# Padding rows issued by one queue instead of two, and 128-column matmuls for half-filled expert tiles

## The chip, the cores and the metric

The kernel runs on one core of a Trainium2 chip. A core has TensorE (matmuls, into PSUM), VectorE, ScalarE, GpSimd and SyncE, each with its own stream of instructions, and 16 DMA engines that serve the queues of SyncE, ScalarE and GpSimd. The engines meet only at semaphores. The metric is the time of one execution on the device, in microseconds.

## The reference

Three stages, each of which takes what the one before gives:

```python
# 1: attention over channels: q, k, v are [2, 5056, 256]
qn = q / (norm(q, axis=1) + 1e-6);  kn = k / (norm(k, axis=1) + 1e-6)
a = softmax(kn.transpose(0, 2, 1) @ qn / tau)          # 256 x 256 per batch
x = (v @ a).reshape(10112, 256)

# 2: mixture of experts, top 1 of E = 8, F = 1024
logits = normalized(x) @ normalized(expert_emb).T / moe_tau
e = argmax(logits);  gate = softmax(logits)[e]
x = gate * (maximum(x @ w1[e], 0) @ w2[e])

# 3: a second one, with its own weights and a second gate
logits = x @ w_gate
e = argmax(logits);  gate = softmax(logits)[e]
out = gate * sigmoid(x @ w_output_gate)[e] * (maximum(x @ w1_b[e], 0) @ w2_b[e])
```

How many tokens an expert gets depends on the data.

## The kernel before

Each of the five engines has one program, written out by hand as a block of the function below.

**Attention.** q and k are loaded in 16 units, TensorE multiplies them (L1116), ScalarE squares them for the norms, whose sums TensorE makes against ones (L1125, L1128). Then v is transposed (L1144) and multiplied with a (L1168), two 128-token slots at a time, with 264 columns: 256 channels and 8 expert logits. VectorE copies the result into `arena` (L847) and works out for every token its expert and its place in that expert's region.

**Dispatch.** GpSimd scatters each row into the DRAM buffer `xbuf[0]` (L503), where expert e has a region of its own from row e·CAP. After the last row of a region there may be old data in the last tile that is read. So `pad_regions` writes 256 pad rows (gate 0, an id that no token has) behind each expert's rows: it loads the expert's count from `plan` (L339) and issues one transfer of 264 KB (L341). There are 8 experts in each of the two layers. SP pads the even experts and ScalarE the odd ones. SP then waits for all scatters (L434, L437) and for all pads (L439), and only then loads the first tile (L443).

**The two expert layers** (m = 0 and 1) run the same loop, `each_tile`, on every engine: over the experts, two at a time, over the full tiles of 256 tokens, and then one tail tile if the count rounded up to 128 is odd. The tail's `subs` is 1, that of a full tile 2. In each tile TensorE does:

- first matrix (L1233): eight chunks c of 128 hidden channels, each 2 × 3 matmuls in reduced-precision fp32 (fp32r): weights are split in a high and a low part, and so is x, and three of the four products are made. The moving operand is x, transposed, with `tok` columns;
- transposes of the next tile's x (L1190);
- second matrix (L1249): per 128 tokens 24 matmuls with 256 columns. It waits for h.

ScalarE evicts each chunk with Relu into `h_hi` (L722) and VectorE makes `h_lo` (L1048), both only over the `subs` × 128 columns that hold tokens. PSUM has four buffers for the chunks. Layer 0 has more in its tiles: TensorE transposes the previous tile's y (L1197), makes its logits (L1204, 16 columns, full fp32) and its ranks (L1210, L1211), VectorE routes it, and GpSimd scatters it into `xbuf[1]`.

The weights of the next expert are split while the current one runs. Where an expert has only a tail tile, the pieces of the split are put between the evictions of that tile: ScalarE's high parts at L624 and L629, VectorE's low parts at L821 and L828, GpSimd's at L520.

Of the tail tile, TensorE's program says before the change:

```python
tok = SUB * P                  # 256, also where subs is 1
... T.matmul(h_ps(c, tok), w1_halves[w][:, par, d, c * P:(c + 1) * P], x_halves[x][:, d, :], ...)
```

so in a tail tile columns 128 to 255 are computed from the rows behind the tile's tokens, and nobody reads them.

Of the kernel before, what the change touches and what calls it, by code (L numbers as in the profile page):

```python
# [28 lines left out]
P = 128  # L29


def build(nc, q, k, v, tau, emb, moe_tau, w1_a, w2_a, w_gate, w_ogate, w1_b, w2_b, out):
    B, N, C = q.shape
    TOK = B * N
    E, _, FF = w1_a.shape
# [14 lines left out]
    SUB = 2  # L50
    PADROWS = SUB * P
    CAP = TOK + PADROWS
# [4 lines left out]
    xbuf = [nc.dram_tensor(f"dispatched_{m}", [E * CAP, ROW], F32, kind="Internal").ap() for m in range(2)]  # L57
# [3 lines left out]
    with ExitStack() as ctx:  # L61
# [19 lines left out]
        pad_rows = sb("pad_rows", [P, SUB, ROW])  # L81
# [93 lines left out]
        plan = [sb(f"plan_{m}", [P, 2, E], I32) for m in range(2)]  # L175
# [19 lines left out]
        def h_ps(c, t):  # L195
            return ps[:, c % HRING, 0:t]
# [48 lines left out]
        padded = [sem(f"padded{m}") for m in range(2)]  # L245
# [87 lines left out]
            eng.dma_start(w1_raw[:, r, :, :], w1_d[m][e]).then_inc(raw_in[r], 16)  # L333
            eng.dma_start(w2_raw[:, r, :, :], w2_d[m][e]).then_inc(raw_in[r], 16)

        def pad_regions(eng, m, first):

            for e in range(first, E, 2):
                count = eng.value_load(plan[m][0:1, 0, e:e + 1], min_val=0, max_val=TOK)  # L339
                dst = xbuf[m][bass.ds(count + e * CAP, PADROWS), :]  # L340
                eng.dma_start(dst.rearrange("(p s) r -> p (s r)", s=SUB), pad_rows[:, :, :].rearrange("p s r -> p (s r)")).then_inc(padded[m], 16)  # L341

        def each_tile(eng, m, before_expert, body, tile, next_weights=None):


# [41 lines left out]
        @block.sync  # L387
        def _(sp):
            def load_group(dst, src, g, signal):

                rows = src[0:FULL * P, :].rearrange("(p t) c -> p t c", t=FULL)
                if g % 2 == 0:
                    sp.dma_start(dst.rearrange("p (t c) -> p t c", c=C), rows[:, g * G:(g + 1) * G, :]).then_inc(signal, 16)
                    return
                body = dst[:, 0:(G - 1) * C].rearrange("p (t c) -> p t c", c=C)
                sp.dma_start(body, rows[:, g * G:(g + 1) * G - 1, :]).then_inc(signal, 16)
                if g < NG - 1:
                    sp.dma_start(dst[:, (G - 1) * C:], rows[:, (g + 1) * G - 1, :]).then_inc(signal, 16)
                else:
                    sp.dma_start(dst[0:REST, (G - 1) * C:], src[FULL * P:N, :]).then_inc(signal, 16)  # L400

            def load_unit(dst, src, j, signal):

                rows = src[0:FULL * P, :].rearrange("(p t) c -> p t c", t=FULL)
                m = U if j < NU - 1 else U - 1
                sp.dma_start(dst[:, 0:m * C].rearrange("p (t c) -> p t c", c=C), rows[:, j * U:j * U + m, :]).then_inc(signal, 16)
                if m < U:
                    sp.dma_start(dst[0:REST, m * C:], src[FULL * P:N, :]).then_inc(signal, 16)

            for n in range(B * NU):  # L410
                b, j = divmod(n, NU)
                if n >= QRING:
                    sp.wait_ge(qk_multiplied, n - QRING + 1)
                    sp.wait_ge(qk_squared, n - QRING + 1)
                load_unit(qk[:, n % QRING, 0, :], q[b], j, qk_in[n % QRING])
                load_unit(qk[:, n % QRING, 1, :], k[b], j, qk_in[n % QRING])
            for n in range(B * NG):
                b, g = divmod(n, NG)
                if n == 2:
                    sp.wait_ge(norm_done, B)  # L420
                    load_weights(sp, 0, 0, 0)
                if n >= 2:
                    sp.wait_ge(vt_done, PAIRS * (n - 1))
                load_group(v_sb[:, n % 2, :], v[b], g, v_in[n % 2])
                if n == 2:
                    load_weights(sp, 0, 1, 1)

            tile = sp.alloc_register("sp_tile")
            for m, L in enumerate(layers):
                sp.wait_ge(plan_ready, m + 1)  # L430
                pad_regions(sp, m, 0)
                if m == 0:
                    for g in range(NG):
                        sp.wait_ge(scattered[g], 16 * G * B)  # L434
                else:
                    n_end = sp.snap(tile)
                    hold(sp, layers[0].y_scattered, n_end * 16 * SUB)  # L437
                    hold(sp, layers[0].xT_ready, n_end + 1)
                sp.wait_ge(padded[m], 16 * E)  # L439

                def load_tile(n, row):
                    hold(sp, L.xT_ready, n)
                    sp.dma_start(x_in[:, :, :], xbuf[m][bass.ds(row, SUB * P), :].rearrange("(s p) r -> p s r", p=P)).then_inc(L.x_in, 16)  # L443

                def body(n, subs, pair, par, t):
                    load_tile(n, pair * (2 * CAP) + par * CAP + t * (SUB * P))

                each_tile(sp, m, lambda *a: None, body, tile)
                load_tile(sp.snap(tile), 0)
            hold(sp, layers[1].y_scattered, sp.snap(tile) * (16 * SUB))  # L450
# [122 lines left out]
        def _(act):  # L573
# [120 lines left out]
            tile = act.alloc_register("act_tile")  # L694
            for m, L in enumerate(layers):
                act.wait_ge(plan_ready, m + 1)
                pad_regions(act, m, 1)
                take_xT(L, 1)

                def before_expert(pair, par, n):  # L700

                    hold(act, w1_split, 2 * pair + (E * m + par + 1))
                    hold(act, w2_split, 2 * pair + (E * m + par + 1))
                    hold(act, w2_split_dve, 2 * pair + (E * m + par + 1))
                    with act.If(pair < E // 2 - 1):
                        load_weights(act, m, nc.s_assert_le(2 * pair + (2 + par), E - 2 + par), par)
                    if m == 0:
                        with act.If(pair > E // 2 - 2):
                            load_weights(act, 1, par, par)

                def ahead(pair, par, n):

                    hold(act, layers[m].tile_done, n)
                    unless_last(act, m, pair, par, lambda: split_w2_hi(pair + (E // 2 * m + par), 1 - par))

                def behind(pair, par, first):
                    unless_last(act, m, pair, par, lambda: split_w1_hi(pair + (E // 2 * m + par), 1 - par))

                def body(n, subs, pair, par, t, splitting=False):
                    for c in range(FC):  # L720
                        act.wait_ge(L.h_done[c], n)
                        nc.scalar.activation(h_hi[:, c, 0:subs * P], h_ps(c, subs * P), ACT.Relu).then_inc(L.h_hi[c], 1)  # L722
                        if m == 0 and c == (3 if subs == 1 else 2):
                            take_yT(n)
                        if splitting:
                            piece = w1_piece if c < WPIECES else w2_piece
                            unless_last(act, m, pair, par, lambda: piece(pair + (E // 2 * m + par), 1 - par, c % WPIECES))
                    take_xT(L, n + 1)
                    if m == 0:
                        y_exps(n)  # L730

                each_tile(act, m, before_expert, body, tile, (ahead, behind))
                if m == 0:
                    n_end = act.snap(tile)
                    take_yT(n_end)
                    y_exps(n_end)
# [345 lines left out]
        def _(pe):  # L1082
            T = nc.tensor
# [132 lines left out]
            for m, L in enumerate(layers):  # L1216
# [6 lines left out]
                    pe.wait_ge(w1_split, pair * 2 + (E * m + par + 1))  # L1223

                def body(n, subs, pair, par, t):
                    tok = SUB * P
                    pe.wait_ge(L.xT_ready, n + 1)
                    for c in range(FC):
                        if c >= HRING:
                            pe.wait_ge(L.h_ready[c - HRING], n)  # L1230
                        for d in range(CC):
                            for at, (w, x) in enumerate(PARTS):
                                last = T.matmul(h_ps(c, tok), w1_halves[w][:, par, d, c * P:(c + 1) * P], x_halves[x][:, d, :],  # L1233
                                                start=(d == 0 and at == 0), stop=(d == CC - 1 and at == len(PARTS) - 1))
                        last.then_inc(L.h_done[c], 1)
                        if m == 0 and c == (2 if subs == 1 else 1):
                            transpose_y(n)
                        if m == 0 and c == (5 if subs == 1 else 4):
                            y_logits(n)
# [46 lines left out]
```

## Time and profile before

| | |
|---|---|
| median of 3 runs | 1494.57 us (1494.0 to 1497.95) |
| the profiled execution | 1497.95 us |
| its span, first to last instruction | 1496.2 us |
| mean granted TensorE clock | 0.934 of full speed |
| tiles | 46 in layer 0, 45 in layer 1 |
| layer 0 / layer 1 begin (first matmul of L1233) | 281.75 / 949.62 us |

TensorE's matmuls overlap: the time that one is shown to last is longer than the distance to the next, so the sum over a group is more than it costs. The clock is 1.00 where TensorE runs at 2.4 GHz and 0.50 where it runs at 1.2 GHz. "PEld" is TensorE's weight load, which goes ahead of each matmul. In the timeline and the chain, an entry with x18 stands for 18 instructions in a row. Full fp32 matmuls appear as two records each, fp32r matmuls and transposes as one.

### The profile page before, as it was taken

Reading aid. Unit: us, or ns where it says so; the run is one execution under the profiler, and the core shown is the slowest. Engines: PE = TensorE matmul, PEld = TensorE weight load, DVE = VectorE, ACT = ScalarE, POOL = GpSimd, SP = SyncE. Lnnn points to the kernel's source line nnn. Section 1 sums busy time; section 2 is a strip of 40 time slices with the busy share of each in tenths; the row PEclk is TensorE's granted clock in tenths of the full one; section 3 lists DMA queues with packets and bytes.
Section 4 is the critical chain, followed back from the end, with each engine's and each line's share of the span. In section 5 each row is a group of like instructions: output and inputs, shape, how many; then the busy total and the mean of one; then the engine's idle time right before and its main releaser. Section 6 shows DMA issues by size and latency. Waiting matters only on the chain.

```text
span 1496.2 us, 30926 instructions
## 1 busy us (share of the span) xinstructions
PE 1327.4 (89%) x10518; PEld 1302.1 (87%) x10519; DVE 805.6 (54%) x2751; ACT 550.5 (37%) x1339; POOL 384.0 (26%) x510
## 2 busy tenths in 40 slices
PE   8978562499999997899999976699999999999985
PEld 7867562499999997899999975699999999999985
DVE  5457455356555567656555566344444544444584
ACT  6547454233333344333333343222333332223362
POOL 1002455312222123312222123222222222222343
PEclk9989686699999998999999987799999999999998
DMA  8635422411111124211111142411111211111260
GB/s 315 244 123 197 142 104 88 156 36 36 43 43 43 36 93 135 82 40 36 43 43 43 36 129 78 144 50 43 43 43 49 94 48 44 48 43 43 96 204 16
DMA packets 68766, 126.20 MB, mean 84 GB/s; under 512 B 9044, under 2 KB 49887, under 8 KB 67712
## 3 DMA queue, kind: packets, MB, share of 16 engines
q1 hardware_dynamic: 35600, 62.57, 13.4%
q10 hardware_dynamic: 20368, 31.55, 6.2%
q0 software_dynamic: 12768, 31.74, 5.9%
q8 instruction: 11, 0.18, 0.1%
q14 instruction: 19, 0.16, 0.0%
HBM read 89.79 MB, written 39.90 MB: 87 GB/s over the span
## 4 chain that ended last, share of the span: by engine, by line
PE 80%; DVE 7%; issue 4%; another core or an unknown queue 2%; ACT 2%; DMA 1%; SPq 1%; DVEq 0%; ACTq 0%; POOL 0%; POOLq 0%
PE ps L1233 35%; PE ps L1249 30%; PE ps L1116 5%; PE ps L1204 3%; PE ps L1190 2%; DVE w_lo L828 2%; PE ps L1168 2%; PE ps L1197 2%; DVE arena L847 1%; DVE h_lo L842 1%; PE ps L1144 1%; ACT w_hi L629 1%; DVE xT_lo L950 0%; DVE w_lo L821 0%
## 5 line engine op out<-in xcount | busy, mean ns | idle before, releaser
L722 ACT ACTIVATE h_hi<-ps 128x256 fp32r<-128x256 f32 (+1 forms) x728 | 268.0, 370 | 694.4 <-PE ps L1233 684.8
L1233 PE MATMUL ps<-xT_hi,w_hi 128*128 128x256 f32 x1456 | 428.1, 294 | 26.2 <-issue 10.8
L1048 DVE SCALAR_TENSOR_TENSOR h_lo<-ps,h_hi 128x256 fp32r<-128x256 f32 (+1 forms) x728 | 294.1, 405 | 245.6 <-ACT h_hi L722 222.6
L1233 PE MATMUL ps<-xT_lo,w_hi 128*128 128x256 f32 x1456 | 415.5, 285 | 0.0
L1233 PE MATMUL ps<-xT_hi,w_lo 128*128 128x256 f32 x1456 | 415.2, 285 | 0.0
L1249 PE MATMUL ps<-w_hi,h_hi 128*128 128x256 f32 x1352 | 393.2, 291 | 0.0
L1249 PE MATMUL ps<-w_lo,h_hi 128*128 128x256 f32 x1352 | 381.8, 282 | 0.0
L1249 PE MATMUL ps<-w_hi,h_lo 128*128 128x256 f32 x1352 | 381.6, 282 | 0.0
L1233 PEld LDWEIGHTS ps<-xT_hi,w_hi 128*128 128x128 f32 x1456 | 284.1, 195 | 30.5 <-issue 17.9
L1233 PEld LDWEIGHTS ps<-xT_hi,w_lo 128*128 128x128 f32 x1456 | 283.2, 194 | 0.0
L1233 PEld LDWEIGHTS ps<-xT_lo,w_hi 128*128 128x128 f32 x1456 | 283.1, 194 | 0.0
L1249 PEld LDWEIGHTS ps<-w_lo,h_hi 128*128 128x128 f32 x1352 | 258.3, 191 | 0.0
L1249 PEld LDWEIGHTS ps<-w_hi,h_lo 128*128 128x128 f32 x1352 | 258.1, 191 | 0.0
L1249 PEld LDWEIGHTS ps<-w_hi,h_hi 128*128 128x128 f32 x1352 | 257.9, 191 | 0.0
L957 DVE COPY y_id<-tag_now 128x2 f32<-128x2 f32 x93 | 24.9, 268 | 235.6 <-PE ps L1249 235.6
L503 POOL DMA_INDIRECT dispatched<-arena,pos_i x80 | 79.3, 991 | 188.2 <-issue 148.4
L503 POOL DMA_INDIRECT dispatched<-y_out,y_pos_i x94 | 93.1, 990 | 57.4 <-POOL y_out L538 42.5
L503 POOL DMA_INDIRECT out_dram<-y_out,y_id_i x92 | 91.9, 999 | 56.1 <-POOL y_out L550 40.5
L1190 PE MATMUL ps<-ident,x_in 128*128 128x128 f32 x372 | 56.7, 275 | 42.9 <-DMA x_in<-dispatched 42.9
L538 POOL COPY y_out<-tag_out 128x4 f32<-128x4 f32 x47 | 9.2, 195 | 332.2 <-DVE y_pos_i L1022 332.2
L549 POOL CAST y_id_i<-y_id 128x2 int32<-128x2 f32 x46 | 8.6, 186 | 311.2 <-DVE y_sb L959 311.2
L1168 PE MATMUL ps<-w_hi,h_hi 128*128 x160 | 54.3, 339 | 31.8 <-DVE arena L847 18.3
(180 smaller groups left out, 1666.3 us busy)
## 6 DMA issues: line engine op xcount, KB each, us to landing
raw<-in_moe_w_dram ACTq DMA_DIRECT2D x28, 1024.0 KB
x_in<-dispatched SPq DMA_DIRECT2D x93, 264.0 KB, 2.8
arena<-in_q_dram SPq DMA_DIRECT2D x14, 640.0 KB, 4.4
arena<-in_k_dram SPq DMA_DIRECT2D x14, 640.0 KB, 5.6
v_sb<-in_v_dram SPq DMA_DIRECT2D x4, 1280.0 KB
v_sb<-in_v_dram SPq DMA_DIRECT2D x4, 1152.0 KB
raw<-in_moe_w_dram SPq DMA_DIRECT2D x4, 1024.0 KB
dispatched<-pad_rows ACTq DMA_DIRECT2D x8, 264.0 KB
```

The costliest lines, as they stand in the source:

```text
L503: pool.indirect_dma_start(dst, bass.IndirectOffsetOnAxis(ap=index, axis=0), src, None, bounds_check=rows - 1, oob_is_err=False).then_inc(s ...
L722: nc.scalar.activation(h_hi[:, c, 0:subs * P], h_ps(c, subs * P), ACT.Relu).then_inc(L.h_hi[c], 1)
L828: return V.tensor_tensor(wpiece(w2_lo, r, i), raw[:, r, W + i * WP:W + (i + 1) * WP], wpiece(w2_hi, r, i), op=ALU.subtract)
L957: V.tensor_copy(y_id[:, :], tag_now[:, :, 1])
L1048: V.scalar_tensor_tensor(h_lo[:, c, 0:subs * P], h_ps(c, subs * P), 0.0, h_hi[:, c, 0:subs * P], op0=ALU.max, op1=ALU.subtract).then_inc(L ...
L1116: last = T.matmul(s_ps(b, c), qk[0:r, j % QRING, 1, t * C + c * P:t * C + (c + 1) * P], qk[0:r, j % QRING, 0, t * C:(t + 1) * C], start=(j ...
L1168: last = T.matmul(x_ps[kk % 2][:, i, :], v_halves[w][:, kk % VRING, i * C + c * P:i * C + (c + 1) * P], a_halves[x][:, bass.ds(b, 1), c, : ...
L1190: last = T.transpose(xt_ps[:, d * SUB * P + s * P:d * SUB * P + (s + 1) * P], x_in[:, s, d * P:(d + 1) * P], ident[:, :])
L1197: last = T.transpose(yt_ps[:, d * SUB * P + s * P:d * SUB * P + (s + 1) * P], y_sb[:, s, d * P:(d + 1) * P], ident[:, :])
L1204: last = T.matmul(lg_ps[:, s, :], yT[:, d, s * P:(s + 1) * P], wg[:, d, :], start=d == 0, stop=d == CC - 1)
L1233: last = T.matmul(h_ps(c, tok), w1_halves[w][:, par, d, c * P:(c + 1) * P], x_halves[x][:, d, :], start=(d == 0 and at == 0), stop=(d == C ...
L1249: last = T.matmul(y_ps[:, s * C:(s + 1) * C], h_halves[h][:, c, s * P:(s + 1) * P], w2_halves[w][:, par, c, :], start=(c == 0 and at == 0) ...
```

## The change

Two edits. The pads of all eight experts are issued by SP alone, for both layers, and ScalarE issues none. And the matmuls of L1233 in a tail tile get 128 columns in place of 256; those of full tiles keep theirs.

```diff
-        def pad_regions(eng, m, first):
-
-            for e in range(first, E, 2):
-                count = eng.value_load(plan[m][0:1, 0, e:e + 1], min_val=0, max_val=TOK)
-                dst = xbuf[m][bass.ds(count + e * CAP, PADROWS), :]
-                eng.dma_start(dst.rearrange("(p s) r -> p (s r)", s=SUB), pad_rows[:, :, :].rearrange("p s r -> p (s r)")).then_inc(padded[m], 16)
...
+            def pad_regions(m):
+
+                for e in range(E):
+                    count = sp.value_load(plan[m][0:1, 0, e:e + 1], min_val=0, max_val=TOK)
+                    dst = xbuf[m][bass.ds(count + e * CAP, PADROWS), :]
+                    sp.dma_start(dst.rearrange("(p s) r -> p (s r)", s=SUB), pad_rows[:, :, :].rearrange("p s r -> p (s r)")).then_inc(padded[m], 16)
+
             tile = sp.alloc_register("sp_tile")
             for m, L in enumerate(layers):
                 sp.wait_ge(plan_ready, m + 1)
-                pad_regions(sp, m, 0)
+                pad_regions(m)
...
                 act.wait_ge(plan_ready, m + 1)
-                pad_regions(act, m, 1)
                 take_xT(L, 1)
...
                 def body(n, subs, pair, par, t):
-                    tok = SUB * P
+                    tok = subs * P
...
-                                last = T.matmul(h_ps(c, tok), w1_halves[w][:, par, d, c * P:(c + 1) * P], x_halves[x][:, d, :],
+                                last = T.matmul(h_ps(c, tok), w1_halves[w][:, par, d, c * P:(c + 1) * P], x_halves[x][:, d, 0:tok],
```

## Rows read from the trace of the kernel before

**Rows 1.** The page's first part: busy time, share of the span, instructions.
```profile
PE 1327.4 (89%) x10518; PEld 1302.1 (87%) x10519; DVE 805.6 (54%) x2751; ACT 550.5 (37%) x1339; POOL 384.0 (26%) x510
```
**Rows 2.** Groups of TensorE by shape: count, busy us and mean ns, idle before.
```profile
L1233 PE MATMUL ps<-xT_hi,w_hi 128*128 128x256 f32 x1456 | 428.1, 294 | 26.2 <-issue 10.8 <-DVE xT_lo L950 7.2 <-DVE w_lo L821 5.0
...
L1233 PEld LDWEIGHTS ps<-xT_hi,w_hi 128*128 128x128 f32 x1456 | 284.1, 195 | 30.5 <-issue 17.9 <-DVE xT_lo L950 8.8 <-DVE h_lo L1048 3.7
```
**Rows 3.** Timeline of TensorE: L1233 at full, then at half clock (start, length).
```profile
289.77 0.28 PE L1233 MATMUL ps<-xT_hi,w_hi 128*128 128x256 f32 x1
...
290.71 0.28 PE L1233 MATMUL ps<-xT_hi,w_lo 128*128 128x256 f32 x1
...
553.32 0.41 PE L1233 MATMUL ps<-xT_hi,w_lo 128*128 128x256 f32 x1
...
555.88 0.41 PE L1233 MATMUL ps<-xT_hi,w_lo 128*128 128x256 f32 x1
```
**Rows 4.** Groups of ScalarE by shape: the evictions of L1233's chunks.
```profile
L722 ACT ACTIVATE h_hi<-ps 128x256 fp32r<-128x256 f32 x624 | 239.1, 385 | 610.3 <-PE ps L1233 609.6 <-issue 0.6
...
L722 ACT ACTIVATE h_hi<-ps 128x128 fp32r<-128x128 f32 x104 | 28.9, 278 | 84.1 <-PE ps L1233 75.2 <-issue 8.8
```
**Rows 5.** The chain of waits through a tile of one expert (start, us).
```profile
552.73 4.21 PE ps L1233 x18
```
**Rows 6.** Stretches of the same tile: length, busy times, then the clock.
```profile
552.00:554.00 2.00, 1.27 (x6) 1.27 (x7) 0.00 (x0) 0.00 (x0) 0.01 (x1) 0.53 0.67 150
...
560.00:562.00 2.00, 2.00 (x20) 2.00 (x19) 1.40 (x4) 1.76 (x5) 0.00 (x0) 1.00 0.03 9
```
**Rows 7.** Timeline of ScalarE in two tail tiles: with weight pieces, and without.
```profile
1464.41 0.28 ACT L722 ACTIVATE h_hi<-ps 128x128 fp32r<-128x128 f32 x1
...
1465.11 0.28 ACT L722 ACTIVATE h_hi<-ps 128x128 fp32r<-128x128 f32 x1
...
1394.18 0.28 ACT L722 ACTIVATE h_hi<-ps 128x128 fp32r<-128x128 f32 x1 [0.43 <-PE ps L1233]
```
**Rows 8.** Chain of waits ahead of layer 1, and a stretch (last: DMA, GB/s).
```profile
935.19 0.37 SPq L341
...
936.33 0.36 SPq L341
...
939.49 3.12 DMA dispatched<-pad_rows
...
944.34 2.57 DMA x_in<-dispatched
...
938.00:940.00 2.00, 0.00 (x0) 0.00 (x0) 0.00 (x0) 0.00 (x0) 0.00 (x0) 0.50 1.01 370
```
**Rows 9.** The chain of waits ahead of layer 0.
```profile
259.20 0.35 SPq L341
...
265.30 8.81 issue
```
**Rows 10.** Timeline of TensorE: L1168, 264 columns, fp32r, full clock.
```profile
211.72 0.28 PE L1168 MATMUL ps<-w_lo,h_hi 128*128 x1
...
212.93 0.28 PE L1168 MATMUL ps<-w_hi,h_lo 128*128 x1
```
**Rows 11.** Timeline of TensorE where few columns stream, and L1204's loads.
```profile
287.70 0.97 PEld L1204 LDWEIGHTS ps<-wg,aT 128*128 128x128 f32 x8
...
46.93 2.42 PEld L1128 LDWEIGHTS ps<-ones,raw 128*128 128x128 f32 x20
...
290.83 0.60 PE L1190 MATMUL ps<-ident,x_in 128*128 128x128 f32 x4
...
928.30 1.78 PEld L1204 LDWEIGHTS ps<-wg,aT 128*128 128x128 f32 x8 [1.09 <-ACT aT L688]
...
L1204 PEld LDWEIGHTS ps<-wg,aT 128*128 128x128 f32 x376 | 46.7, 194 | 1.1 <-ACT aT L688 1.1
```
**Rows 12.** Timeline of TensorE: L1116, 256 columns in full fp32.
```profile
28.62 4.70 PE L1116 MATMUL ps<-arena 128*128 128x256 f32 x21
```

## The prediction

> **What bounds the kernel now.** I read the page's head first: TensorE is busy 89% of the span, no other engine above 54% [rows 1]. The profiled execution took 1497.95 us, of which 1496.2 us is the span and 1.75 us lies around it; it is the slowest of the three runs, 3.4 us above their median of 1494.57. My sum is a difference made in the trace, and I carry it over to the median.
>
> The groups of TensorE say where the time lies: the largest is that of L1233, an expert's first matrix, whose matmuls last 294 ns [rows 2]; five more like it follow (two more parts of L1233, three of L1249, the second matrix). 294 ns is how long one lasts, not how often one starts. For that one goes to the timeline: eight steps of L1233 take from 289.77 to 290.71, so one starts every 0.1175 us at full clock; at half clock 12 steps take 553.32 to 555.88, 0.2133 us each [rows 3]. I call this the step.
>
> Which tiles does the change touch? The evictions of L1233 have two shapes: 624 of 256 columns and 104 of 128. At 8 per tile that is 78 full tiles and 13 half tiles [rows 4]. A half tile has 8 × 6 = 48 matmuls at L1233, so 13 × 48 = 624 matmuls go from 256 to 128 columns.
>
> What sets the end in such a tile? The chain of waits through one that is an expert's only tile shows TensorE first (4.21 us for its first 18 matmuls, and some 5 us more to its last), then ScalarE's evictions and weight pieces, then VectorE's weight pieces [rows 5]. By the stretches, the clock there starts at 0.50 and is at 1.00 by 560, some 7 us later [rows 6]. ScalarE, alternating an eviction and a weight piece, needs 1464.41 to 1465.11, 0.70 us per chunk [rows 7]; TensorE at full clock needs 6 × 0.1175 = 0.705. They are level.
>
> The second place is the pause ahead of each of the two expert layers. Ahead of the second, ScalarE's and SP's queues issue four pads each, side by side, SP's from 935.19 to 939.49; the DMA engines are full meanwhile (share 1.01, 370 GB/s) and no compute engine does anything; the last pad lands 3.12 us after its issue, at 942.61, and the next x_in leaves at 944.34 [rows 8]. The chain of waits runs through these rows, so the pads are on the path. Ahead of the first layer the pads are not: SP has issued its last by 265.30 and then waits 8.81 us, to 274.11, for GpSimd's row scatters [rows 9].
>
> **The change, part by part.**
>
> *Pads on SP alone, second layer.* SP issues 8 instead of 4; ScalarE issues none, but it then only waits for the transposes, which wait for x_in, so its freed time buys nothing. SP's first two issues are 1.14 us apart (935.19, 936.33), the next two 1.58 on average, while the DMA engines are full [rows 8]. One queue offers 264 KB per 1.14 us or about 230 GB/s, under the 370 GB/s seen there, so I take little growth. Bounds: the eighth issue at 935.19 + 7 × 1.14 = 943.2, or, by the widest mean spacing (1.92, ahead of the first layer, below), at 948.6. It lands after 2.57 us (an x_in of the same 264 KB on idle queues) to 3.12: 945.7 to 951.7. Against 942.61 now that is +3.1 to +9.1 us. I take +3.5, near the low end, since the growth came with full DMA engines. Behind these issues on SP stand the wait for the scatters, the wait for the pads and x_in's load; TensorE, ScalarE and VectorE wait for that.
>
> *Pads on SP alone, first layer.* The wait for the scatters covers it. At the spacing above, the eighth issue is at 259.20 + 7 × 1.14 = 267.2, and landed by 269.8; at the mean spacing seen here (first issue at 259.20, the fourth ended at 265.30 after 0.35 us, so (264.95 − 259.20)/3 = 1.92) it is at 272.6 and lands at 275.2 to 275.8, after 274.11 [rows 9]. So 0 to +1.7; I take 0. Were the scatters not there, it would cost as in the second layer.
>
> *128 columns for 256.* No row has a reduced-precision (fp32r) matmul of 128 columns. Two things can set its step. The streaming of columns: with 264 columns ten steps take 211.72 to 212.93, 0.121 us each, so 8 columns more cost about 3.5 ns [rows 3, 10]; 128 fewer would take off 56 ns, to 0.062. And the weight load: where next to nothing streams, steps do not get short. 8 loads beside 16-column matmuls take 0.97 us, (0.97 − 0.19)/7 = 0.111; 20 loads beside 1-column matmuls take 2.42, (2.42 − 0.19)/19 = 0.117; four transposes of 128 columns take 0.60, (0.60 − 0.275)/3 = 0.108; at half clock the 16-column ones take (1.78 − 0.33)/7 = 0.207 [rows 11]. Those are fp32 operands, and fp32r could load faster; but the load of an fp32r matmul lasts 195 ns, and that of the fp32 ones 194 [rows 2, 11]. So I take 0.111 at full clock and no change at half clock: 6.5 ns off a matmul.
>
> The Trainium skill (TensorE: Matmul & The Clock Gate, "LDWEIGHTS (loading the stationary operand)") has a load take its columns over 1.2 GHz, 107 ns for 128: by it the halved columns bring at most 10 ns a matmul, an estimate; these loads' steps of 108 to 117 ns agree.
>
> What is exposed of it: ten of the 13 half tiles are an expert's only tile, and by ScalarE's timeline weight pieces ride along in them; there ScalarE's 0.70 us per chunk lies level with TensorE, which at 6 × 0.111 = 0.67 gains next to nothing. The other three (two behind full tiles, and the last tile of all) have no pieces, and ScalarE waits 0.43 us for TensorE at each chunk [rows 7]; there about 48 × 6.5 ns = 0.3 us each. I take −1 us in all; bounds are 0 and, if everything were exposed at 0.108, 624 × 9.5 ns = −6.
>
> Sum: +3.5 + 0 − 1 = **+2.5 us**; 1497.95 becomes 1500.5, and the median 1494.57 becomes **1497.1**. Own range of this case: −6 + 3.1 = −3 to 9.1 + 1.7 = +10.8 us, 1491.6 to 1505.4.
>
> **The rivals.**
>
> *A. Streaming decides (faster).* If fp32r weights load fast enough, the step is 0.062 us at full clock and 56 × 2 = 0.11 less than now at half clock. In the seven tiles of the first layer, of which six start at half clock, some 18 matmuls save 0.11 each, 2 us, and ScalarE's 0.70 is then the bound. The three tiles without pieces save 48 × 0.056 = 2.7 each, the three others of the second layer some 0.5: 12 + 8 + 2 = −22, with the pads −18: 1476. For it: the slope of 264 against 256 columns [rows 10]. Against: every step with few columns in rows 11. It decides below a step of some 0.10. The Trainium skill (TensorE: Matmul & The Clock Gate, "Back-to-back issue gap") gives about 81 ns for a stream of 128-column matmuls with their loads; that would bring some two thirds of this gain, and no run here shows it.
>
> *B. Short matmuls fall back to full fp32 (slower).* Full fp32 takes two records a matmul (20 for the ten matmuls of L1128 [rows 11]), and 21 records of 256 columns take 4.70 us, 0.22 each [rows 12]: 0.45 us a matmul against 0.1175. If 128 columns were handled so, two records of 0.108 to 0.117 make 0.22 to 0.23, +0.11 us for each of 624 matmuls, all exposed as TensorE becomes the bound: +65 us, and with the pads 1563. For it: nothing in the trace; against it: nothing either, as no fp32r matmul there has under 256 columns. The Trainium skill (FP8 and Floating Point Precision, "TensorE Precision Notes") tells the one pass of reduced fp32 from the four of true fp32, and says nothing of columns.
>
> *C. The clock stays low (slower).* In the only-tile experts the clock comes back within about 7 us of dense 256-column matmuls [rows 6]; whether it does with 128 no row shows. If not, the remaining 30 matmuls cost 0.207 to 0.213 for 0.1175, +2.8 us, and the 8 records of the logits 1.78 for 0.97 [rows 3, 11]: up to +4 in six tiles, and +4.6 in those of the second layer if they drop too: +20 to +50, middle 1530. For it: half clock already shows in these tiles. Against it: TensorE stays without gaps there in any case, as the steps hardly change.
>
> **How the numbers follow.** Within 0.3% (4.5 us, about what a measurement of this kernel tells from no change) I call the same. My case holds 0.46 (same 0.35, slower 0.10, faster 0.01); A 0.14, faster; B 0.20, slower; C 0.15, slower; the rest, 0.05, is slower spacing of pads than bounded or something unseen (same 0.01, slower 0.03, faster 0.01). Together: faster 0.16, same 0.36, slower 0.48. Slower has the most chance though the likeliest single case is "same", since both bad mechanisms lie on that side. Range: 1482 leaves out about half of A, 1552 leaves out the most of B: together about 2 in 10. The likeliest case's own range is 1491.6 to 1505.4.
>
> **What would show it.** Steps of L1233 in a half tile: 0.111 at full clock (mine), 0.062 (A), 0.22 with two records (B), 0.207 over a whole tile with the clock at 0.50 (C). For the pads: eight issues of SP between 935 and 944, x_in leaving 3.5 us later relative to the plan's end; the same ahead of the first layer without delay. It would be wrong if the count's load grew on a lone queue, or if fp32r at 128 columns took another path than rows 2 and 11 let me see.

## The result, and the profile after

| | median, us | runs |
|---|---|---|
| before | 1494.57 (1494.0 to 1498.82) | 5 |
| after | 1512.11 (1506.4 to 1516.06) | 5 |

The ratio is 1.0105, with a 95% interval of 1.0076 to 1.0134: by the ratio 15.7 us slower, and 17.5 between the medians. That is inside the stated range and on the side that had the most chance, but it is not the case that was held for the likeliest (+2.5 us). It is rival C, the clock, as the rest shows. After the change the times of single executions also lie further apart, 10 us in place of 5. The profiled execution of the changed kernel took 1505.39 us, one of its quickest, 7.4 us more than that of the kernel before. It enters the first expert layer 3.1 us earlier (278.69 for 281.75), since the scatters ahead of it end 3.1 us earlier (271.06 for 274.11), and no run shows whether the change has a part in that; from there to the end it is 10.5 us longer.

Busy times and shares of the changed kernel, and the granted clock in 40 slices:

```profile
PE 1344.7 (89%) x10518; PEld 1320.5 (88%) x10519; DVE 802.1 (53%) x2751; ACT 553.7 (37%) x1339; POOL 384.1 (26%) x510
...
PEclk9988786799999986999999976799999999999987
```

TensorE is busy 17 us longer [rows 1] though it streams fewer columns, with the same number of instructions. L1233 is now L1232. Its groups by shape:

```profile
L1232 PE MATMUL ps<-xT_hi,w_lo 128*128 128x256 f32 x1248 | 349.3, 280 | 0.0
...
L1232 PE MATMUL ps<-xT_hi,w_hi 128*128 128x128 f32 x208 | 69.6, 335 | 16.7 <-issue 8.8 <-DVE xT_lo L949 4.2 <-DVE w_lo L820 3.7
L1232 PE MATMUL ps<-xT_hi,w_lo 128*128 128x128 f32 x208 | 69.5, 334 | 0.0
```

3 × 208 = 624 matmuls have 128 columns, as counted. One record each, so they are not run as full fp32. But a short one lasts 335 ns on average and a long one 280: at 0.28 us each at full and 0.41 at half clock (below), some four in ten of the short ones ran at half clock. The timeline gives the steps at either clock:

```profile
862.60 0.28 PE L1232 MATMUL ps<-xT_lo,w_hi 128*128 128x128 f32 x1
...
864.39 0.27 PE L1232 MATMUL ps<-xT_hi,w_lo 128*128 128x128 f32 x1
...
553.13 0.42 PE L1232 MATMUL ps<-xT_lo,w_hi 128*128 128x128 f32 x1
...
556.55 0.41 PE L1232 MATMUL ps<-xT_hi,w_lo 128*128 128x128 f32 x1
```

Between the first two lie 16 steps, 1.79/16 = 0.112 us at full clock; between the last two 16 as well, 3.42/16 = 0.214 at half clock. Half the columns take 5% off the step at full clock and nothing at half clock [rows 3]. The Trainium skill (TensorE: Matmul & The Clock Gate, "LDWEIGHTS (loading the stationary operand)") has a load take its columns over 1.2 GHz, by which 128 columns are 107 ns, an estimate. The 0.112 of full clock agrees to 5%; at half clock the step is 0.214, twice that, and there the measurement decides.

Now the only-tile experts, by stretches (length, busy times of PE, PEld, DVE, ACT, POOL, then clock, DMA share, GB/s):

```profile
552.00:554.00 2.00, 2.00 (x12) 2.00 (x11) 1.60 (x4) 1.18 (x3) 0.85 (x1) 0.50 0.98 396
...
560.00:562.00 2.00, 2.00 (x11) 2.00 (x11) 0.94 (x6) 1.52 (x4) 1.03 (x1) 0.50 0.00 0
562.00:564.00 2.00, 2.00 (x11) 2.00 (x11) 2.00 (x2) 0.66 (x2) 1.93 (x2) 0.50 0.00 0
564.00:566.00 2.00, 2.00 (x13) 2.00 (x11) 1.68 (x11) 0.22 (x1) 0.00 (x0) 0.60 0.00 0
```

Before, the clock was back at 1.00 by 560 in such a tile [rows 6]. Now this tile starts at 550.00, behind a pause of 2.19 us, and its first 18 matmuls still run at full clock (the last starts at 551.95). Then the clock falls to 0.50, and it stays there through the rest of the first matrix. It comes up only at about 565.5, well into the 256-column matmuls of L1248, which start at 561.75.

The next tile, before and after, in the chain of waits:

```profile
570.45 4.21 PE ps L1233 x18
...
587.50 4.20 PE ps L1233 x18
```
```profile
568.35 3.51 PE ps L1232 x18
571.86 0.87 PE ps L1196 x4
572.73 3.73 PE ps L1232 x18
576.46 1.63 PE ps L1203 x8
578.09 2.65 PE ps L1232 x12
...
587.39 2.22 PE ps L1232 x18
```

Its 48 matmuls of the first matrix, by the timeline from the start of the first to the end of the last, take 12.4 us (568.35 to 580.73) and took 9.8 (570.45 to 580.23); its distance to the next tile went from 17.05 to 19.04 us.

The pads, in the chain of waits ahead of the second layer, and then ahead of the first:

```profile
937.54 0.37 SPq L426
...
938.67 0.36 SPq L426
...
945.80 2.04 DMA dispatched<-pad_rows
...
949.59 2.72 DMA x_in<-dispatched
```
```profile
264.95 0.18 SPq L426
...
271.06 0.03 SPq L434
```

SP's eight issues are (945.80 − 937.54)/7 = 1.18 us apart, and the last lands at 947.84. From the first issue to x_in's load it is 12.05 us; it was 9.15 [rows 8]: +2.9. Ahead of the first layer SP has issued its last pad at 264.95 and the scatters end at 271.06, 6 us later: hidden, as before [rows 9]. While the eight pads of the second layer are issued, the DMA engines move 237 GB/s (938 to 940, share 0.64) and 215 (940 to 942, share 0.58), where two queues had them full at 370 [rows 8].

### The profile page after: what moved, and what is told of

The parts are those of the page before. It is cut to its first block, busy times and chain, and to the rows that moved or that the text cites. A ratio compares the mean times of both kernels' runs of the same rounds, so it can differ in the third digit from the quotient of the medians.

```text
span 1503.7 us, 30926 instructions
## 1 busy us (share of the span) xinstructions
PE 1344.7 (89%) x10518; PEld 1320.5 (88%) x10519; DVE 802.1 (53%) x2751; ACT 553.7 (37%) x1339; POOL 384.1 (26%) x510
## 4 chain that ended last, share of the span: by engine, by line
PE 81%; DVE 7%; issue 4%; another core or an unknown queue 2%; ACT 2%; SPq 1%; DMA 1%; ACTq 1%; DVEq 0%; POOL 0%; POOLq 0%
PE ps L1232 35%; PE ps L1248 30%; PE ps L1115 5%; PE ps L1203 3%; PE ps L1189 3%; PE ps L1167 2%; PE ps L1196 1%; DVE w_lo L827 1%; DVE arena L846 1%; PE ps L1143 1%; ACT w_hi L629 1%; DVE h_lo L841 1%; SPq L424 1%; DVE w_lo L820 0%
## 5 line engine op out<-in xcount | busy, mean ns | idle before, releaser
L1232 PE MATMUL ps<-xT_hi,w_hi 128*128 128x256 f32 (+1 forms) x1456 | 428.5, 294 | 27.0 <-issue 9.9
L1232 PE MATMUL ps<-xT_hi,w_lo 128*128 128x256 f32 (+1 forms) x1456 | 418.8, 288 | 0.0
L1232 PE MATMUL ps<-xT_lo,w_hi 128*128 128x256 f32 (+1 forms) x1456 | 418.5, 287 | 0.0
L1248 PE MATMUL ps<-w_hi,h_hi 128*128 128x256 f32 x1352 | 399.1, 295 | 0.0
L1248 PE MATMUL ps<-w_lo,h_hi 128*128 128x256 f32 x1352 | 386.7, 286 | 0.0
L1248 PE MATMUL ps<-w_hi,h_lo 128*128 128x256 f32 x1352 | 386.1, 286 | 0.0
L1232 PEld LDWEIGHTS ps<-xT_hi,w_hi 128*128 128x128 f32 x1456 | 287.7, 198 | 31.5 <-issue 17.1
L1232 PEld LDWEIGHTS ps<-xT_hi,w_lo 128*128 128x128 f32 x1456 | 287.9, 198 | 0.0
L1232 PEld LDWEIGHTS ps<-xT_lo,w_hi 128*128 128x128 f32 x1456 | 287.3, 197 | 0.0
L1248 PEld LDWEIGHTS ps<-w_lo,h_hi 128*128 128x128 f32 x1352 | 263.9, 195 | 0.0
L1248 PEld LDWEIGHTS ps<-w_hi,h_hi 128*128 128x128 f32 x1352 | 263.8, 195 | 0.0
L1248 PEld LDWEIGHTS ps<-w_hi,h_lo 128*128 128x128 f32 x1352 | 263.2, 195 | 0.0
L1189 PEld LDWEIGHTS ps<-ident,x_in 128*128 128x128 f32 x372 | 45.2, 149 | 44.3 <-issue 44.3
```

What stands on the lines that cost most here:

```text
L1189: last = T.transpose(xt_ps[:, d * SUB * P + s * P:d * SUB * P + (s + 1) * P], x_in[:, s, d * P:(d + 1) * P], ident[:, :])
L1248: last = T.matmul(y_ps[:, s * C:(s + 1) * C], h_halves[h][:, c, s * P:(s + 1) * P], w2_halves[w][:, par, c, :], start=(c == 0 and at == 0) ...
```

## The experiments

They ran on three other chips (runs 1 to 4, 5 to 8, 9 to 11), on which the kernel before takes 1452.7 to 1453.7 us. Each is compared with runs of the kernel before on its own chip. Changes in us below are the ratio times its time.

**1. The pads alone.** The changed kernel, with this:

```diff
-                    tok = subs * P
+                    tok = SUB * P
...
-                                last = T.matmul(h_ps(c, tok), w1_halves[w][:, par, d, c * P:(c + 1) * P], x_halves[x][:, d, 0:tok],
+                                last = T.matmul(h_ps(c, tok), w1_halves[w][:, par, d, c * P:(c + 1) * P], x_halves[x][:, d, :],
```

> Only the pads are moved: SP issues all eight in both layers, and the half tiles keep 256 columns. Clock theory (the half columns cost the time, the pads 3 us): the first tile of the second layer leaves about 3 us later after its plan than before (10.1 us from plan to load becomes 13), nothing ahead of the first layer, and the whole is +3 us, 1497.5, ratio 1.002. Pad theory (the single queue is the cause of the whole loss): +12 to +16 us, ratio 1.010.

Measured: 1.0018 (1.0010 to 1.0027), +2.6 us. Its chain of waits has the same picture as that of the changed kernel, 12.05 us from the first issue to x_in:

```profile
893.18 0.37 SPq L426
...
901.44 2.04 DMA dispatched<-pad_rows
905.23 2.71 DMA x_in<-dispatched
```

**2. The columns alone.** The kernel before, with this:

```diff
-                    tok = SUB * P
+                    tok = subs * P
...
-                                last = T.matmul(..., x_halves[x][:, d, :],
+                                last = T.matmul(..., x_halves[x][:, d, 0:tok],
```

> Only the columns are changed: 128 in the half tiles, pads as before on two queues. Clock theory: the steps are 0.109 us at full and 0.207 at half clock, the clock is at 0.50 through most of the half tiles that are an expert's only tile, and the whole is +9 to +14 us, ratio 1.006 to 1.009, with a wider spread between executions than the kernel before has. Pad theory: no loss, ratio 1.000 or a little under.

Measured: 1.0100 (1.0069 to 1.0131), +14.5 us, single executions from 1457.5 to 1475.3. Within their intervals the two parts add up to the change. A tile of an only-tile expert runs at half clock from its first to its last chunk, by stretches:

```profile
516.00:520.00 4.00, 4.00 (x21) 4.00 (x21) 2.18 (x7) 2.38 (x6) 0.61 (x1) 0.50 1.04 393
...
524.00:528.00 4.00, 4.00 (x20) 4.00 (x21) 0.57 (x5) 1.32 (x5) 0.58 (x1) 0.50 0.02 4
```

**3. 192 columns.** Is it the columns that keep the clock low, or the step that the weight load bounds? With 192 columns the step is still bound by the load.

```diff
-                    tok = SUB * P
+                    tok = SUB * P if subs == SUB else 192
...
-                                last = T.matmul(..., x_halves[x][:, d, :],
+                                last = T.matmul(..., x_halves[x][:, d, 0:tok],
```

> The kernel before with 192 columns in the half tiles (64 of them computed and not read). Theory that the columns streamed decide on the clock: the step is the weight load's 0.109 us as with 128, but the clock comes back and stays, so the time is that of the kernel before or 1 us under it, ratio 0.999 to 1.001. Rival, that it is the step bound by the weight loads that keeps the clock low: it stays low as with 128 columns, ratio 1.005 to 1.009. By streaming alone (no load bound) the step would be 0.092.

Measured: 1.0006 (0.9996 to 1.0016). The loss is gone. Stretches and steps of one tile:

```profile
534.00:536.00 2.00, 2.00 (x14) 2.00 (x14) 1.60 (x4) 1.30 (x3) 0.17 (x1) 0.63 0.98 354
536.00:538.00 2.00, 2.00 (x21) 2.00 (x19) 1.20 (x4) 1.61 (x5) 0.00 (x0) 1.00 1.05 376
```
```profile
535.63 0.27 PE L1233 MATMUL ps<-xT_lo,w_hi 128*128 128x192 f32 x1
...
537.42 0.28 PE L1233 MATMUL ps<-xT_hi,w_lo 128*128 128x192 f32 x1
```

16 steps in 1.79 us, 0.112 each, exactly those of 128 columns; but the clock comes back as with 256. So the rival falls: a step bound by the load does not by itself hold the clock down. And 64 columns fewer bring nothing that shows in the time.

**4. All matmuls of the first matrix cut to 128 columns**, in the kernel before:

```diff
-                        for d in range(CC):
-                            for at, (w, x) in enumerate(PARTS):
-                                last = T.matmul(h_ps(c, tok), ..., x_halves[x][:, d, :], ...)
+                        for half in range(subs):
+                            for d in range(CC):
+                                for at, (w, x) in enumerate(PARTS):
+                                    last = T.matmul(h_ps(c, SUB * P)[:, half * P:(half + 1) * P], ...,
+                                                    x_halves[x][:, d, half * P:(half + 1) * P], ...)
```

> The kernel before with every L1233 matmul cut to 128 columns: full tiles run each chunk as two halves of six matmuls, so 96 matmuls for 48, half tiles 48 of 128. It measures step and clock of 128-column matmuls over a long stretch without pauses. If the clock stays full in dense work whatever the columns: 96 x 0.109 = 10.5 us for 5.64 in 78 tiles, +380 us. If 128 columns pull the clock down even there: 96 x 0.207 = 19.9 us and the rest of the tile partly at half clock too, +1100 us or more. If the clock goes back and forth with the 256-column matmuls of L1249 in between: between the two.

Measured: 1901.44 us in one execution, +449. By stretches, two in one full tile of the first layer and one where the only-tile experts lie, and by the timeline of that tile:

```profile
402.00:404.00 2.00, 2.00 (x21) 2.00 (x19) 0.95 (x3) 0.38 (x1) 1.70 (x2) 1.00 0.19 68
...
412.00:414.00 2.00, 2.00 (x21) 2.00 (x19) 1.23 (x7) 0.38 (x1) 0.00 (x0) 1.00 0.00 0
...
640.00:700.00 60.00, 54.32 (x297) 53.27 (x297) 35.24 (x121) 21.27 (x53) 19.81 (x20) 0.64 0.38 124
```
```profile
402.17 0.28 PE L1234 MATMUL ps<-xT_lo,w_hi 128*128 128x128 f32 x1
...
404.62 0.28 PE L1234 MATMUL ps<-xT_hi,w_lo 128*128 128x128 f32 x1
```

22 steps take 2.45 us, 0.111 each. From 402 to 414 TensorE runs no matmul of more than 128 columns, and the clock is 1.00 all along. So in dense work 128 columns do not pull down a clock that is up. Where the only-tile experts lie, with their pauses (640 to 700), it is 0.64. The same run has the opposite case in its very first tile, by the chain of waits:

```profile
242.20 5.38 PE ps L1234 x24
...
257.66 7.76 PE ps L1234 x36
...
266.30 5.07 PE ps L1251 x27
```

The clock is at 0.50 when this tile starts and at 0.50 in every stretch to 270: all 96 matmuls of 128 columns, with transposes and the logits among them, run without a pause from 242.20 to 265.4 and leave it there, 23 us, and it comes back between 270 and 272, in the 256-column matmuls behind them. The program is the same as from 402 to 414.

The steps alone make 96 × 0.1114 = 10.7 us for 5.64 in 78 tiles, +395. Of the other 54 us some 35 lie in the four full tiles that begin behind a pause (at 242.20, 684.12, 1138.28 and 1784.52): they are 44 us longer than full tiles in dense work, and in the trace of the kernel before such tiles are 9 us longer. The half tiles, which cost 14.5 us in run 2, are in the rest.

**5 and 6. Half of the chunks.** If short matmuls only fail to bring back a fallen clock, the order of short and long ones in the tile must matter. Both have 128 columns in half of the chunks of a half tile; this is run 5, and run 6 has `c >= 4` in it:

```diff
-                    tok = SUB * P
...
                     for c in range(FC):
...
+                        tok = SUB * P if subs == SUB or c < 4 else P
...
-                                last = T.matmul(..., x_halves[x][:, d, :],
+                                last = T.matmul(..., x_halves[x][:, d, 0:tok],
```

> The kernel before, where in a half tile the chunks 0 to 3 keep 256 columns and the chunks 4 to 7 get 128. Theory (128-column matmuls do not bring the clock back once it is down, but do not pull it down either when it is up): the clock comes back during the first four chunks as before and stays up, so the time is that of the kernel before, ratio 0.998 to 1.002. Rival (fewer columns pull the clock down by themselves): half clock in the second half and in the matmuls behind it, ratio 1.004 or more.

> The reverse: chunks 0 to 3 of a half tile get 128 columns and chunks 4 to 7 keep 256; as many columns in all as in the run before. Theory: the clock stays at half through the first four chunks and comes back only in the second half, so most of the loss is there, +6 to +12 us, ratio 1.004 to 1.008. Rival (the sum of the columns in a tile decides): the same as the run before.

Measured: run 5 1.0006 (0.9997 to 1.0014), run 6 1.0074 (1.0061 to 1.0087), +10.8 us. The same columns in all, in another order. Stretches of the second half tile, first run 5, then run 6:

```profile
534.00:536.00 2.00, 2.00 (x18) 2.00 (x17) 1.49 (x3) 1.19 (x5) 0.00 (x0) 0.88 0.96 300
...
538.00:540.00 2.00, 2.00 (x20) 2.00 (x20) 1.24 (x8) 1.80 (x5) 0.43 (x1) 1.00 0.62 223
```
```profile
536.00:538.00 2.00, 2.00 (x11) 2.00 (x11) 0.93 (x3) 1.64 (x5) 0.00 (x0) 0.50 1.05 377
538.00:540.00 2.00, 2.00 (x14) 2.00 (x12) 1.14 (x3) 1.24 (x3) 0.60 (x1) 0.60 0.37 130
540.00:542.00 2.00, 2.00 (x19) 2.00 (x19) 0.58 (x5) 1.08 (x4) 0.10 (x2) 1.00 0.00 0
```

In run 5 the first four chunks, with 256 columns, bring the clock back and it stays up under the 128-column ones behind them (538 to 540). In run 6 it comes back only when the 256-column chunks have begun. With the same sum of columns, the order makes the difference between +0.06% and +0.74%.

**7. TensorE kept busy over the pauses** of the first layer's half tiles with matmuls of constants, whose results nobody reads; 256 columns in the half tiles, pads as before:

```diff
+                def keep_busy(count):
+                    for i in range(count):
+                        T.matmul(h_ps(0, P), ones[:, :], ident[:, :], start=True, stop=True)
...
                             if m == 0 and s * FC + c == 4 + 2 * subs:
+                                if subs == 1:
+                                    keep_busy(8)
                                 y_rank(n)
                         if s == subs - 1:
                             last.then_inc(L.tile_done, 1)
+                    if m == 0 and subs == 1:
+                        keep_busy(7)
```

> The kernel before (256 columns, pads on two queues), and in the half tiles of the first layer TensorE gets 8 full-fp32 matmuls of constants ahead of the wait for the ranks and 7 behind its last matmul, whose results are not read: about 1.7 and 1.5 us that fill most of its pauses of 2.3 and 1.8 us. If the pauses are what lets the clock fall: the next tile starts at full clock and five tiles save up to 2.5 us each, -5 to -12 us, ratio 0.992 to 0.997. If the clock falls all the same or the added work delays the ranks: 1.000 to 1.003.

Measured: 0.9938 (0.9925 to 0.9951), −9.0 us: by the ratios faster than both kernels. The tile behind a filled pause starts at full clock, by the stretch around its start at 530.56 and by the chain, where the first 18 matmuls of the tile after that take 2.26 us; in such tiles they took 4.21 [rows 5]:

```profile
530.00:532.00 2.00, 1.64 (x14) 1.46 (x14) 1.19 (x5) 0.14 (x1) 0.57 (x2) 1.00 0.68 168
```
```profile
545.31 2.26 PE ps L1237 x18
```

**8. The same with 128 columns.** Run 7, with the edit of run 2.

> The run before with 128 columns in the half tiles. Theory (128 columns only fail to bring a fallen clock back): with the clock kept up over the pauses they cost little; the loss against the run before is under half of the 15 us that the columns cost without the filler. Rival (128 columns cost the clock in any case): the full +12 to +16 us against the run before.

Measured: 1.0005 (0.9989 to 1.0021); against run 7 that is 1.0005/0.9938 = 1.0067, some 9.7 us. I had expected less than half of 15, so this missed. The stretches say where the rest is:

```profile
522.00:526.00 4.00, 4.00 (x21) 4.00 (x21) 0.92 (x3) 1.32 (x5) 0.00 (x0) 0.50 0.00 0
...
536.00:541.00 5.00, 5.00 (x47) 5.00 (x47) 3.26 (x11) 3.96 (x11) 1.57 (x2) 1.00 0.96 338
```

The first line is the half tile that starts at 513.97, behind the longer pause that follows full tiles, which has no filler. Its clock falls and 128 columns leave it down to the end. The second is the next one, behind filler: it stays at 1.00 with 128 columns. Both kinds of tile behave as the theory has it; what I misjudged is how many tiles the filler reaches. The two half tiles of the first layer without it are 5.3 and 3.8 us longer than in run 7 (21.90 for 16.57 us to the next tile, and 20.39 for 16.57), 9.1 of the 11.3 us between the two profiled executions (1456.48 and 1445.15).

**9 to 11. Half the pad rows.** 128 rows are enough behind an expert if a half tile loads only its own 128:

```diff
-                dst = xbuf[m][bass.ds(count + e * CAP, PADROWS), :]
-                eng.dma_start(dst.rearrange("(p s) r -> p (s r)", s=SUB), pad_rows[:, :, :].rearrange("p s r -> p (s r)")).then_inc(padded[m], 16)
+                dst = xbuf[m][bass.ds(count + e * CAP, P), :]
+                eng.dma_start(dst, pad_rows[:, 0, :]).then_inc(padded[m], 16)
...
-                    sp.dma_start(x_in[:, :, :], xbuf[m][bass.ds(row, SUB * P), :].rearrange("(s p) r -> p s r", p=P)).then_inc(L.x_in, 16)
+                    sp.dma_start(x_in[:, 0:subs, :], xbuf[m][bass.ds(row, subs * P), :].rearrange("(s p) r -> p s r", p=P)).then_inc(L.x_in, 16)
```

Run 9 is this on the kernel before, run 10 on run 1 (all on SP), run 11 on run 7.

> The kernel before with 128 pad rows behind each expert in place of 256 (132 KB a transfer), and with the load of a half tile cut to its 128 rows, so that nothing unwritten is read. If the DMA engines' bytes set the pause ahead of the second layer (1.08 MB in place of 2.16 at 370 GB/s is 2.9 us less, but four issues 1.14 us apart on each queue take 3.8 us): -1.5 to -2.5 us, ratio 0.998 to 0.999. If the issues alone set it: no difference.

> All pads on SP as in the run with only the pads moved, and they are of 128 rows. Theory that eight issues in a row set the end of the pads on one queue: the spacing of the issues stays 1.1 us and the last lands only a few tenths sooner, so +1.5 to +2.5 us against the kernel before, ratio 1.001 to 1.002. Theory that the bytes of the single queue set it: the halves bring the 2.6 us back, ratio 1.000 or under.

> The kernel with the filler matmuls and 256 columns, with the half-size pads on two queues. The gains add up if both theories hold: -9.7 for the filler and about -2 for the pads, ratio 0.992, as far as the measurement tells.

Measured: run 9 0.9979 (0.9970 to 0.9988), −3.1 us; run 10 1.0010 (1.0000 to 1.0019), +1.5; run 11 0.9920 (0.9907 to 0.9934), −11.6. Chains of waits of run 9, then of run 10:

```profile
892.77 0.35 SPq L341
...
896.26 1.89 DMA dispatched<-pad_rows
899.88 2.64 DMA x_in<-dispatched
```
```profile
891.44 0.36 SPq L426
...
899.56 1.75 DMA dispatched<-pad_rows
903.05 2.75 DMA x_in<-dispatched
```

On two queues the issues now come (896.26 − 892.77)/3 = 1.16 us apart in place of 1.43, and x_in leaves 7.11 us after the first issue in place of 9.15: with the full pads the bytes of both queues together held the issues up. On one queue half the bytes change nearly nothing: 1.16 for 1.18 apart, 11.61 us for 12.05 to x_in. There eight issues in a row are the time. Run 9 also halves the loads of the half tiles, and no run parts that from the pads: x_in's earlier start is 2.0 us of its 3.1. Run 11 is the best version found: 1441.17 us where the kernel before takes 1453.57.

## Why the prediction was right or wrong, point by point

- **Pads ahead of the second layer, +3.5 (bounds +3.1 to +9.1).** Measured +2.9 in the trace and +2.6 (1.5 to 3.9) by run 1. The spacing of 1.14 was seen as 1.18, so the reason was right: a lone queue does not fill the DMA engines (215 to 237 GB/s). What was a little high is the last landing, 2.04 us where 2.57 to 3.12 was taken.
- **Pads ahead of the first layer, 0.** Right: SP waits another 6 us for the scatters behind its last issue (271.06 against 264.95).
- **The step of a 128-column matmul, 0.111 at full and unchanged at half clock.** Right: 0.112 and 0.214. Rival A (0.062, or the 81 ns that stand beside it) and rival B (two records, 0.22) fall with it, and run 3 shows the same floor at 192.
- **The clock.** This is the step that failed. The own case let it be as it was, and against rival C the prediction put that "TensorE stays without gaps there in any case". It does, and the clock stays down all the same. The rows of a tile at both clocks were there [rows 5, 6], but they told only that the clock comes back under 256 columns; that it would under 128 too was assumed, at a cost of nothing in the sum. Runs 2, 3, 5 and 6, and the first tile of run 4, show that here it does not: +14.5 us with 128 columns alone, nothing measurable with 192. That the result still lies in the stated range is not to the credit of the likeliest case, whose own range ended at 1505.4; the range was wide enough to hold C, which had 0.15.
- **The size of rival C, +20 to +50 for an actual +14.5.** Its term for a first-layer tile, up to +4 in six tiles, was too large. In the tile at 568.35 the first matrix grows by 2.6 us (12.4 for 9.8) and the distance to the next by 2.0 (19.04 for 17.05), as VectorE's two weight pieces behind it take 2.70 us in place of 3.29; in the tile at 874.05 the distance grows by 2.7 (20.06 for 17.39). Others grow less: those at 550.00 and 587.39 by 0.6 and 0.8 (18.35 for 17.72, 17.87 for 17.11), and the one at 894.11 is 1.5 us shorter than before (15.38 for 16.83). And the tiles of the second layer did not all drop: in the profiled execution the clock fell in two of the last ones, and from the half tile at 1432.82 to the end it is 3.7 us longer.
- **−1 us for the short step.** Too small to be seen; runs 3 and 5, where the clock holds, are at 1.0006 and do not show a gain. The trace does show the term where nothing hides it: the half tile behind full tiles takes 13.93 us to the next one (860.12 to 874.05) and took 14.30 (860.05 to 874.35), 0.37 for the 0.3 that was said.

What is not settled: why the clock is up behind a pause in one tile or execution and not in another (the tile at 894.11 of the changed kernel starts with 18 matmuls in 2.22 us and keeps 1.96 for the next 18, its neighbours take 3.73), which may be what spreads the times. In that tile the clock then falls at about 900.1, 6 us behind the pause, while 128-column matmuls run without a gap. So what run 4 shows of dense work is not shown for a tile behind a pause. One profiled execution can't tell.

## What to carry to other kernels

In this kernel, where each matmul has its own weight load, one of 128 columns has the same step as one of 192 (0.112 us at full clock) and gains only 5% on one of 256. Columns that nobody reads cost next to nothing there, and with them the clock came back after a pause. Look in the trace for stretches at half clock that follow TensorE's pauses before shortening the matmuls there, or fill the pause with matmuls of constants, which gave 9 us here. And splitting work over two queues paid here because on one queue eight issues in a row set the end, and not the bytes: with half the bytes the issues of one queue stay as far apart (1.16 us for 1.18), those of two queues draw closer (1.16 for 1.43).

## What was not expected of the hardware

- In run 4 the 96 short matmuls of a full tile, without a pause among them, ran at 1.00 from their first to their last in dense work (12 us, 402 to 414) and at 0.50 from their first to their last where the clock was down at their start (23 us, 242 to 265).
- The kernel before took 1452.7 to 1453.7 us on the three other chips and 1494.6 on the first. In run 3, whose profiled execution took 1453.30 us, the first matmul of the first expert layer comes at 244.0, and at 281.75 in the 1497.95 us of the kernel before on the first chip: 38 of the 45 us lie in the stages ahead of it. No run here tells why.
- VectorE's two weight pieces take 3.29 us where GpSimd's start 0.25 us ahead of them (563.35 and 563.10 before), and 2.69 where they start 0.81 us ahead (561.78 and 560.97 after). That they slow each other down is an inference from this, and no run parts them.
